# Clustered attention with two MoE blocks: a pair's two heads interleaved slot by slot, P normalised before the transposes, x split straight from PV's banks

## The reference

```
q_assign = argmax(q_n @ c_n); k_assign = argmax(k_n @ c_n)
scores   = where(q_assign[:, None] == k_assign[None, :], (q @ k.T) / sqrt(D), -1e9)
attn     = exp(scores - max(scores)); attn = attn / (sum(attn) + 1e-9)
x        = attn @ v                               # heads side by side: (1536, 512)
x        = ((x @ w1) * (x @ w2) @ w3) @ w_out     # d_ff 1024
h        = x @ w_in                               # d_ff 2048
out      = (h * clip(h + 3, 0, 6) / 6) @ w_out2
```

## Time and profile before

| what | value |
|---|---|
| median of 3 runs | 792.84 us |
| profiled execution | 791.82 us |
| its span | 790.0 us |
| PE busy | 759.5 us (96%) |
| DVE busy | 420.9 us (53%) |
| ACT busy | 340.8 us (43%) |
| POOL busy | 303.8 us (38%) |
| share of PE in the chain that ended last | 85% |

### The profile page before, as it was taken

The page is one execution under the profiler, slowest core; times in us unless marked ns, Lnnn a source line. Parts: engine busy times, 40 slices in busy tenths (PEclk is TensorE's granted clock), DMA queues, the critical chain, the costliest instruction groups (busy, mean ns, idle before and its releaser), DMA issues.

```text
span 790.0 us, 11968 instructions
## 1 busy us (share of the span) xinstructions
PE 759.5 (96%) x3809; PEld 579.9 (73%) x3809; DVE 420.9 (53%) x556; ACT 340.8 (43%) x644; POOL 303.8 (38%) x278
## 2 busy tenths in 40 slices
PE   6898999999999999999999999979999999999996
PEld 4676666666666666888788878868888788878885
DVE  5115666666665663654644465544544545454552
ACT  6225666676676674423323233233333333343332
POOL 4862324423432301332423243324544444444541
PEclk9999999999999999999999999999999999999999
DMA  8543464456445411121221121212323423242221
GB/s 304 141 134 105 106 145 122 108 117 150 103 110 132 102 33 47 55 79 53 65 67 54 53 80 53 67 53 82 104 95 104 144 82 106 93 146 96 90 93 53
DMA packets 41457, 77.55 MB, mean 98 GB/s; under 512 B 6096, under 2 KB 11216, under 8 KB 41424
## 3 DMA queue, kind: packets, MB, share of 16 engines
q1 hardware_dynamic: 39696, 73.98, 32.7%
q10 hardware_dynamic: 1728, 3.15, 1.0%
HBM read 53.51 MB, written 3.15 MB: 72 GB/s over the span
## 4 chain that ended last, share of the span: by engine, by line
PE 85%; POOL 4%; issue 3%; DVE 2%; ACT 2%; DMA 2%; SPq 1%; ACTq 1%; DVEq 0%; POOLq 0%
PE ps L766 19%; PE ps L768 18%; PE ps L767 18%; PE ps L873 10%; PE ps L860 8%; PE ps L848 5%; PE ps L850 4%; POOL b_lo L334 2%; DMA wo_raw<-in_wo 1%; PE ps L818 1%; ACT out_sb L562 1%; PE ps L892 1%; DVE g_lo L735 1%; PE ps L883 1%; POOL qk_split L358 1%
## 5 line engine op out<-in xcount | busy, mean ns | idle before, releaser
L334 POOL TENSOR_TENSOR b_lo<-stage,b_hi 128x512 fp32r<-128x512 f32 x160 | 213.1, 1341 | 328.9 <-ACT b_hi L330 328.9
L766 PE MATMUL ps<-x_hi,b_hi 128*128 (+1 forms) x384 | 149.9, 390 | 0.0
L768 PE MATMUL ps<-x_hi,b_lo 128*128 (+1 forms) x384 | 149.4, 389 | 0.0
L767 PE MATMUL ps<-x_lo,b_hi 128*128 (+1 forms) x384 | 149.4, 389 | 0.0
L330 ACT CAST b_hi<-stage 128x512 fp32r<-128x512 f32 x160 | 95.9, 619 | 94.3 <-PE ps L768 77.5
L662 DVE TENSOR_REDUCE neg_max<-ps 128x1 f32<-128x768 f32 x96 | 91.2, 951 | 26.7 <-PE ps L850 26.6
L759 DVE SCALAR_TENSOR_TENSOR gate<-side,ps 128x512 f32<-128x512 f32 x48 | 33.0, 687 | 125.4 <-ACT side L549 125.1
L449 ACT ACTIVATE probs<-ps,neg_max 128x768 f32<-128x768 f32 x96 | 86.8, 904 | 25.3 <-DVE neg_max L662 25.3
L733 DVE CAST g_hi<-gate 128x512 fp32r<-128x512 f32 x72 | 94.6, 1314 | 2.5
L768 PEld LDWEIGHTS ps<-x_hi,b_lo 128*128 128x128 f32 x384 | 72.1, 188 | 15.0
L767 PEld LDWEIGHTS ps<-x_lo,b_hi 128*128 128x128 f32 x384 | 72.1, 188 | 14.8
(11 more groups left out here) (84 smaller groups left out, 913.1 us busy)
## 6 DMA issues: line engine op xcount, KB each, us to landing
stage<-in_wio SPq DMA_DIRECT2D x96, 256.0 KB, 2.9
stage<-in_w SPq DMA_DIRECT2D x64, 256.0 KB, 3.0
qk_ops<-qk_split SPq DMA_DIRECT2D x32, 384.0 KB, 4.8
qk_raw<-in_qk SPq DMA_DIRECT2D x16, 384.0 KB, 5.0
qk_ops<-qk_split SPq DMA_DIRECT2D x32, 192.0 KB, 4.6
v_raw<-in_v SPq DMA_DIRECT2D x16, 192.0 KB, 2.3
out<-out_sb ACTq DMA_DIRECT2D x12, 256.0 KB, 2.9
wo_raw<-in_wo SPq DMA_DIRECT2D x8, 256.0 KB, 5.8
```

Source lines behind the costliest of these rows:

```text
L334: nc.gpsimd.tensor_tensor(b_lo[par][:, halves[half]], stage[par][:, halves[half]], b_hi[par][:, halves[half]].bitcast(F32), ALU.subtract). ...
L766: nc.tensor.matmul(psum, w_hi, m_hi, start=start, stop=False)
L767: nc.tensor.matmul(psum, w_hi, m_lo, start=False, stop=False)
L768: return nc.tensor.matmul(psum, w_lo, m_hi, start=False, stop=stop)
```

## The change

- **Slots interleaved.** Slot s is now tile 0, 1 or 2 of the pair's first head, then the same of its second head, then tiles 3 to 5 of the first, then of the second (`slot`). Six slots are a *unit*: half of the queries, of both heads.
- **PV.** A unit's PV puts the first head's 64 features in the lower and the second head's in the upper partitions of one bank. That is already x with features on partitions. Units take turns on banks 6 and 7, so `pv_rows`, `head_out`, `normalize` and `x_columns` are gone; `x_high` and `x_low` read the PV bank.
- **Normalisation.** DVE takes the reciprocal of each slot's sums by itself (`reciprocal`, two operations of one column per slot), and POOL multiplies P, 128x768, in place (`normalise`, once per slot). Transposes of slot s wait for that and not for the exponential; they are issued one slot later (loop step s issues `score(s + 2)`, `transposes(s - 1)`, then PV). P has four buffers, not three.
- **The ring** has two banks, 4 and 5, and so `next_use` waits for use k - 2. `logits`, `logit_columns` and `hot` of head n stand where `prepared` puts them: after the PV of steps s = 2, 4 and 0 (mod 6), that is after the transposes of tiles 1, 3 and 5 of a unit.
- **DVE's order.** In a step it does reciprocal(s), `row_max(s + 2)`, and then the group copies of slot s - 1 (before: copies of slot g, then `row_max(g + 2)`). `best_rank` with the multiplication that was POOL's `rank_hot` stands between the reciprocal and `row_max` of one step in six.
- **POOL's order** is now one normalisation per slot with one piece of preparation behind it (`split_lo` in two halves).
- **Start and end.** `logits(2)` and `logit_columns(2)` move into the fold stretch, `best_of(2)` and `best_rank(2)` stand ahead of `row_max(0)`, and `hot(2)` ahead of the first transposes. The last unit's PV (12 matmuls) is issued within the first `up`, at its step 2.
- v has four buffers, and its loads and the others are reordered to suit.

```
-PV, ACC = 6, 4
-RING_BANKS = (4, 5, 7)
+ACC = 4
+RING_BANKS, PV_BANKS = (4, 5), (6, 7)
...
+def slot(s):
+
+    unit, r = divmod(s, ST)
+    return unit // 2 * 2 + r // 3, unit % 2 * 3 + r % 3
...
+def prepared(s):
+
+    n, step = divmod(s + AHEAD, ST)
+    return (n + 2 if n + 2 < HEADS else None), step
...
+    uses = [(use, n) for use in ("logits", "cols", "hot") for n in range(2)] + [("logits", 2), ("cols", 2)]
+    for s in range(SLOTS + 1):
+        if s >= 1:
+            unit, i = divmod(s - 1, ST)
+            uses += [("probs", unit * GROUPS + j // GROUP) for j in range(ST * i, ST * i + ST) if j % GROUP == 0]
+        n, step = prepared(s)
+        if n is not None and step in (1, 3, 5):
+            uses.append((("logits", "cols", "hot")[step // 2], n))
...
+            def normalise(s):
+                pool.wait_ge(s_recip, s + 1)
+                nc.gpsimd.tensor_scalar(probs[s % PROBS][:], probs[s % PROBS][:], recips[:, s:s + 1], 1.0,
+                                        ALU.mult, ALU.mult).then_inc(s_norm, 1)
...
+            for s in range(SLOTS):
+                normalise(s)
+                n, step = prepared(s)
+                if n is not None:
+                    if step == 0:
+                        scale_q(n)
+                    if step == 1:
+                        split_hi(n)
+                    if step in (2, 3):
+                        split_lo(n, step - 2)
+                    if step == 4:
+                        hot_columns(n)
...
-            def x_high(k):
-                use = ("x", k)
-                act.wait_ge(s_fill[ring_bank(use)], ring_turn(use) + 1)
-                nc.scalar.copy(x_hi[:, x_cols(k)], ring(use)[:, 0:HALF]).then_inc(s_xh, 1)
-
-            def pv_rows(n):
-                act.wait_ge(s_pv, n + 1)
-                if n >= 2:
-                    act.wait_ge(s_fill[ring_bank(("out", n - 2))], ring_turn(("out", n - 2)) + 1)
-                nc.scalar.copy(pv_out[n % 2][:], ps[:, PV, 0:HALF]).then_inc(s_ev, 1)
+            def x_high(unit):
+                act.wait_ge(s_pv, unit + 1)
+                nc.scalar.copy(x_hi[:, x_cols(unit)], ps[:, PV_BANKS[unit % 2], 0:HALF]).then_inc(s_xh, 1)
...
+            def reciprocal(s):
+                dve.wait_ge(s_exp, s + 1)
+                step(nc.vector.tensor_scalar(sums1[:, s:s + 1], sums[:, s:s + 1], 1e-9, None, ALU.add))
...
+                nc.vector.reciprocal(recips[:, s:s + 1], sums1[:, s:s + 1]).then_inc(s_recip, 1)
...
+            for s in range(SLOTS + 1):
+                if s < SLOTS:
+                    reciprocal(s)
+                n, step_of = prepared(s)
+                if n is not None and step_of == 4:
+                    best_rank(n)
+                if s + 2 < SLOTS:
+                    row_max(s + 2)
+                if s >= 1:
+                    unit, i = divmod(s - 1, ST)
+                    for k in groups_of(s - 1):
...
+                    if i == ST - 1 and unit >= 1:
+                        x_low(unit - 1)
+                if n is not None and step_of == 3:
+                    best_of(n)
...
-                for h in range(2):
-                    first = 3 * h * ST + t
-                    mm = nc.tensor.matmul(ps[h * D:(h + 1) * D, PV, 0:HALF].rearrange("p (a b) -> p a b", a=3),
-                                          v_raw[n % 2][:, t, :], probs_t[:, n % 2, first:first + 2 * ST + 1:ST, :],
...
+                for side in range(2):
+                    first = 3 * side * ST + t
+                    mm = nc.tensor.matmul(ps[side * D:(side + 1) * D, PV_BANKS[unit % 2], 0:HALF].rearrange("p (a b) -> p a b", a=3),
+                                          v_raw[(unit // 2 * 2 + side) % 4][:, t, :],
+                                          probs_t[:, unit % 2, first:first + 2 * ST + 1:ST, :],
...
+            for s in range(SLOTS + 1):
+                if s + 2 < SLOTS:
+                    score(s + 2)
+                if s >= 1:
+                    transposes(s - 1)
+                if s >= ST + 1:
+                    p_times_v(*divmod(s - 1 - ST, ST))
+                n, step = prepared(s)
+                if n is not None and step in (1, 3, 5):
+                    (logits, logit_columns, hot)[step // 2](n)
```

More of the change, by code:

```diff
@@ L35, with last_slot @@
 DVE_GROUPS = (1, 4, 7)
-PV, ACC = 6, 4
-RING_BANKS = (4, 5, 7)
+ACC = 4
+RING_BANKS, PV_BANKS = (4, 5), (6, 7)
+UNITS = HEADS
+AHEAD = 5
+PROBS = 4
 FOLD = (2, 6)
 SETS = 4
-def ring_order():
[L44 to L58, removed]
+def slot(s):
+    unit, r = divmod(s, ST)
+    return unit // 2 * 2 + r // 3, unit % 2 * 3 + r % 3
+def last_slot(n):
+    return n // 2 * 2 * ST + ST + n % 2 * 3 + 2
+def prepared(s):
+    n, step = divmod(s + AHEAD, ST)
+    return (n + 2 if n + 2 < HEADS else None), step
+def ring_order():
+    uses = [(use, n) for use in ("logits", "cols", "hot") for n in range(2)] + [("logits", 2), ("cols", 2)]
[6 more added lines that the diff above has]
+            uses.append((("logits", "cols", "hot")[step // 2], n))
     return uses
@@ new lines, in _ @@
+            for s in range(SLOTS + 1):
+                if s + 1 < SLOTS:
+                    exp(s + 1)
+                if s >= 1:
+                    unit, i = divmod(s - 1, ST)
+                    for k in groups_of(s - 1):
+                        if k % GROUPS not in DVE_GROUPS:
+                            use = ("probs", k)
+                            if unit >= 2:
+                                act.wait_ge(s_pv, unit - 1)
+                            act.wait_ge(s_fill[ring_bank(use)], ring_turn(use) + 1)
+                            at = k % GROUPS * GROUP
+                            nc.scalar.copy(probs_t[:, unit % 2, at:at + GROUP, :].rearrange("p a b -> p (a b)"), ring(use)
+                                           ).then_inc(s_rel[ring_bank(use)], 1)
+                    if i == ST - 1 and unit >= 1:
+                        x_high(unit - 1)
+                n, step = prepared(s)
+                if n is not None and step == 1:
+                    rows_of_logits(n)
+                if n is not None and step == 5:
+                    mask_rows(n)
+                if s == SLOTS - 2:
+                    act.wait_ge(s_scores, last_slot(HEADS - 2) + 1)
@@ L654, in best_rank @@
             def best_rank(n):
-                dve.wait_ge(s_ranked, n + 1)
+                use = ("cols", n)
+                dve.wait_ge(s_rel[ring_bank(use)], ring_turn(use) + 1)
                 if n >= 1:
                     dve.wait_ge(s_diff, n)
+                step(nc.vector.tensor_tensor(hot1[:], hot0[:], rank[:], ALU.mult))
+                own.wait()
                 nc.vector.tensor_reduce(best2[:], hot1[:], AX.X, ALU.max).then_inc(s_b2, 1)
@@ L837, in hot, with score @@
                 mm.then_inc(s_fill[ring_bank(("hot", n))], 1)
-            def score(g):
-                n, i = divmod(g, ST)
+            def score(s):
+                n, i = slot(s)
                 if i == 0:
```

297 lines of the change are left out of this document (101 added, 196 removed).

## The result

| | before | change |
|---|---|---|
| median, us | 792.60 (791.52 to 794.27, 8 runs) | 796.14 (793.90 to 799.12, 8 runs) |
| ratio to before | | 1.0044, 95% interval 1.0023 to 1.0066 |
| profiled execution, us | 791.82, span 790.0 | 794.34, span 792.5 |

The change makes the kernel slower by about 3.5 us in the medians and by 2.5 us between the two traces. The forecast was 799 us, with 791 to 809 as its range: right in sign and range, 2.9 us too high (a loss of 6.2 us was forecast, one of 3.5 measured).

A forecast was written before the change was run, and what follows sets the result against it. PE was taken to bound attention, busy for all 40 us of each window. The terms -7.4 + 13.0 - 0.9 + 4.6 - 3.1 = +6.2 us, added to 792.84, gave 799 us, range 791 to 809.

The forecast's parts named there:

- output transposes gone from the loop: PE, slots 6 to 93: 25 `head_out` and `x_columns` at 0.295 us each go, -7.4 us.
- stalls at the preparations: PE beside PV: three waits per head for DVE's late group copy, 12 heads, 0.36 us each, +13.0 us.
- one set of preparations moved to the start: Loop: head 2's preparations move ahead, and all others with them, so one set leaves the stretch, -0.9 us.
- start: Up to slot 6's transposes: later first row maximum and uncovered copies in the first unit, 82.8 instead of 78.21, +4.6 us.
- end: After slot 93: six output transposes, 0.67 us idle and some 0.6 of late exponentials go, -3.1 us.
- The mechanism: Preparations beside PV: two ring banks make PE wait for DVE's copy, queued behind a row maximum; chance of this theory 0.60.
- X: The start of a step's transposes on PE; without a stall a preparation may follow at 1.55 us after it.
- the time from a release to the waiting matmul: From the end of DVE's group copy to PE's preparation matmul: taken as 0.15 us.
- part case: Rival: a stall of 0.15 to 0.25 us, or a cheaper start, ends within 2.4 us of before; chance 0.11.
- Hidden, as said: Attention: reciprocals (0.4 us a slot), POOL's normalisation (80 us in all) and loads were to cost PE nothing.
- DVE and POOL blocking each other: Rival, step after `best_of`: POOL's normalisation holds a DVE ranking operation, 9 us more, 808 us; chance 0.12.
- The covered bank wait: Rival, preparations: row maximum and copy don't stand in PE's way, only removals count, -10 us, 783 us; chance 0.14.

The follow-up runs named there:

- e1: The changed kernel with three ring banks (4, 5, 7) and one bank (6) for PV: 784.73 us, ratio 0.9896.
- e2: The changed kernel, two ring banks, with DVE's group copies ahead of the row maximum of the same step: 785.42 us, ratio 0.9900.
- e3: The changed kernel with DVE copying groups 2, 5, 8 and ACT the others, including those the preparations meet: 784.97 us, ratio 0.9896.
- e8: The changed kernel with one small, untied DVE operation added ahead of the wait in each of its group copies: 799.22 us, ratio 1.0075.
- e9: The changed kernel with two one-column DVE operations, each waited for, ahead of each DVE group copy: 812.13 us, ratio 1.0258.
- e5: The three-bank version with head 2's columns in mid last fold and its best_of and best_rank ahead of DVE's last fold copy: 782.74 us, ratio 0.9867.
- e7: The changed kernel, two ring banks, with only the start reordered as in e5: 794.44 us, ratio 1.0019.
- e4: The changed kernel without POOL's 96 normalising multiplications; transposes wait for the exponential instead: 794.71 us, ratio 1.0033.
- e6: The three-bank version with the second score computed three times, keeping PE busy longer before its pause: 783.34 us, ratio 0.9891.

## Why the prediction came out as it did

The sum, step by step, on the two profiled executions:

| step | predicted, us | by the trace of the change, us |
|---|---|---|
| output transposes gone from the loop | -7.4 | -7.4 (period = 14.98 and three stalls) |
| stalls at the preparations | +13.0 (36 x 0.36) | +9.4 (36 x 0.26) |
| one set of preparations moved to the start | -0.9 | -0.9 |
| one score moved out of the loop | not in the sum | -0.8 (a score of the earlier trace rows) |
| start | +4.6 | +4.85 |
| end | -3.1 | -2.74 |
| sum | +6.2 | +2.4 (the spans: +2.5) |

- **The mechanism was right**, to the operation: DVE's copy stands behind a row maximum that can't start before X + 0.20, the bank ring of two makes each preparation wait for it, 36 times, and it ends at X + 1.76. `e1` to `e3` take it away in three ways, `e8` and `e9` add to it, and each moves the period by the amount of the stall. That the time lies in the range says less: 791 to 809 us also holds the kernel before.
- **The size was off by one term: the time from a release to the waiting matmul.** I took 0.15 us out of one row, where POOL's `hot_columns` releases PE. Behind DVE's copy it was 0.05: the copy ends at 202.46 + 0.68 = 203.14, and the matmul starts at 203.19. So the stall was 0.26 and not 0.36, and 36 x 0.10 = 3.6 us too many came of it. The other deviations (-0.8, +0.25, +0.36) nearly cancel. The "part case" put a stall of 0.15 to 0.25 us within 2.4 us of before; the measured stall lies at its edge, and so does the result (2.5 us between the spans, 3.5 between the medians). The trace of before had both values of the release, and two rows of its timeline (POOL and PE) show the small one for POOL:

```profile
29.92 0.82 POOL L346 TENSOR_SCALAR qk_raw<-qk_raw 64x768 f32<-64x768 f32 x1
30.79 0.63 PE L818 MATMUL ps<-qk_raw,cent_t 128*32 128x256 f32 x6 [2.42 <-POOL qk_raw L346]
```

From POOL's end at 30.74 to the matmul at 30.79 pass 0.05 us. Behind DVE's `g_lo` there it is 0.14 (521.19 + 1.63 to 522.96) and 0.06 (616.79 + 1.65 to 618.50). So the engine alone doesn't set it. With 0.05 the forecast's stall would have been 0.26 and its sum +2.6 us; I used the larger of the two values that the trace held.

- **A term was missed.** With transposes one slot later, `score(3)` stands ahead of the first transposes. I counted it in the start (68.3) but did not take it out of the stretch from slot 6 to slot 93: after the change slot 93's transposes follow slot 92's by 306.78 - 305.24 = 1.54 us, with no score between. The loop's sum is then -7.4 - 0.9 + 9.4 - 0.8 = +0.3, and 0.43 was measured.
- **Start and end.** First transposes at 68.84 (68.3 forecast), slot 6 at 83.06 (82.8). The row maximum came at 65.07 and not at 64.4: `logit_columns` for head 2 stood behind the whole last fold and `best_of` behind DVE's last fold copy (it began at 63.63; the forecast's 64.4 less four operations of 0.36 is 62.96). `e5` and `e7` move just that. The end gave 2.74 of 3.1.
- **Hidden, as said**: POOL's normalisation in the changed kernel (`e4`), the reciprocals (0.14 and 0.16 us) and the loads. In the change no wait of PE from 85 to 306 us is for anything but the copy.
- **DVE and POOL blocking each other** did not come. At that place DVE was first, 0.18 us ahead of POOL (204.54 and 204.72), its operation took 0.36 us as without the normalisation, and POOL's took 0.95 where the ones beside nothing took 0.91. That is the order I had argued; what POOL first would have cost was not tried. By the rule that the forecast quoted from the Trainium skill ("SBUF — State Buffer", section "SBUF: two separate sides") POOL's would have started its work only at DVE's end, at 204.90, and been 0.18 us longer; the row shows 0.04 longer. Spans on POOL are rough, and so this neither bears the rule out nor contradicts it.
- **The covered bank wait**, 783 us with a chance of 0.14, was not what the change does. It is what `e1` to `e3` do: 784.7 to 785.4 us.
- **Median and trace.** The medians differ by 3.5 us and the traces by 2.5, since the profiled execution is one of the change's two with the highest mean clock.

## What to carry to other kernels

Ask of each shared buffer not how many there are but which operation frees the one that comes next, and what its engine does just ahead of it. Here the whole gain of the restructuring (7.4 us of PE's work) was taken back by one copy that stood behind one reduction, and one constant, `DVE_GROUPS`, or the order of two calls gave it back. On an engine that is busy for all of a loop, a wait of a quarter of a microsecond that recurs 36 times is the change; read who releases, and where the rows give two values for the release (here 0.05 and 0.15 us), carry both through the sum: over 36 waits they are 3.6 us apart.

## What the runs showed of the hardware

- **From a release to PE's waiting matmul it is 0.05 to 0.06 or 0.13 to 0.15 us**, by the profile's modelled ends, and neither value belongs to one engine: 0.05 to 0.06 behind DVE's group copy (in `e9` too, 206.64 + 0.69 to 207.38), ACT's exponential (65.34 + 0.19 to 65.58 in the kernel before) and POOL's `scale_q`; 0.14 to 0.15 behind POOL's `hot_columns` and ACT's `pv_rows` (306.69 + 0.48 to 307.31); DVE's `g_lo` shows both. What decides was not found.
- **The same shape is not the same price on POOL**: 128x768 times a number per row took 0.91 us, the multiplication by a constant 0.835. The two differ in the type of their target as well, and no run parts these.
- **Two DVE operations that don't depend on each other overlap**: the copy started 0.06 us after a one-column operation of 0.14. Where DVE waited for its own result, the next started 0.18 us later.
- **The clock can fall with a pause of 2.5 us** that interrupts full work: to 0.50 of full speed, for 3.4 or 6.8 us, in five traces of seven, at a price of 2.05 us in the one pair that isolates it. Elsewhere it fell once in eleven times at 1.8 to 1.9 us and never at 1.7 or less. Computing something useless in the pause (`e6`) was cheaper than pausing in these two traces; the medians don't prove it.
